# Hashed attention ahead of two feed-forward layers: sign bits laid by DMA below the features of the second score product, scores copied under a ceiling

## What is computed

```python
q_bits = (np.einsum('bhsd,dk->bhsk', q, proj) > 0)
k_bits = (np.einsum('bhsd,dk->bhsk', k, proj) > 0)
mask = q_bucket[:, :, :, None] == k_bucket[:, :, None, :]
scores = np.where(mask, scale * np.matmul(q, k.transpose(0, 1, 3, 2)), -1000000000.0)
attn = np.exp(scores - np.max(scores, axis=-1, keepdims=True))
attn = attn / (np.sum(attn, axis=-1, keepdims=True) + 1e-09)
out = np.matmul(attn, v)
```

## Time and profile before

| | us |
|---|---|
| median of 3 runs | 783.49 (781.36 to 784.22) |
| profiled execution | 782.37 |
| its span, first to last instruction | 780.6 |
| PE busy | 763.5 (98%) |
| DVE busy | 405.1 (52%) |
| ACT busy | 343.6 (44%) |
| POOL busy | 288.9 (37%) |
| granted TensorE clock, mean | 0.999 |

### The profile page before, as it was taken

How to read it: one execution, slowest core, us unless ns; L and a number is a source line. 1 busy time by engine, 2 the same in 40 slices (tenths; PEclk the granted TensorE clock), 3 DMA queues, 4 the chain that set the end, 5 groups by cost and what they waited for, 6 DMA issues and landing times.

```text
span 780.6 us, 12163 instructions
## 1 busy us (share of the span) xinstructions
PE 763.5 (98%) x3800; PEld 644.7 (83%) x3800; DVE 405.1 (52%) x688; ACT 343.6 (44%) x657; POOL 288.9 (37%) x230
## 2 busy tenths in 40 slices
PE   7999999999999999999999999999999999999998
PEld 6788888888889888888888888888888888888886
DVE  5888887888898574343333432352323333242333
ACT  7988898888987221232212322132221312222121
POOL 3688878878897493000000366660000000000000
PEclk9999999999999999999999999999999999999999
DMA  6576667666762342000000032310001000010001
GB/s 168 136 148 167 146 141 177 151 127 157 157 120 61 84 136 82 1 0 1 1 0 1 27 100 89 107 55 0 1 1 42 11 0 0 0 54 0 0 0 54
DMA packets 46312, 52.77 MB, mean 68 GB/s; under 512 B 8912, under 2 KB 34768, under 8 KB 46288
## 3 DMA queue, kind: packets, MB, share of 16 engines
q1 hardware_dynamic: 46064, 52.13, 27.0%
q10 hardware_dynamic: 224, 0.33, 0.2%
HBM read 32.73 MB, written 3.19 MB: 46 GB/s over the span
## 4 chain that ended last, share of the span: by engine, by line
PE 75%; DMA 8%; POOL 6%; issue 5%; SPq 3%; DVE 2%; ACT 0%; POOLq 0%; DVEq 0%
PE acc L594 33%; PE h_ps L576 32%; DMA inv_dram<-row_inv 4%; DMA all_inv<-inv_dram 3%; PE pt_ps L542 2%; POOL wa_lo L431 2%; POOL kt L385 2%; PE pv_ps L556 2%; PE pv_ps L557 1%; PE s_ps L528 1%; PE s_ps L529 1%; POOL wa_hi L429 1%; POOL pt_hi L395 1%; DMA w_raw<-w_out_dram 1%; DVE w_raw L837 1%
## 5 line engine op out<-in xcount | busy, mean ns | idle before, releaser
L770 ACT ACTIVATE r_sb<-h_ps 128x512 f32<-128x512 f32 x96 | 57.4, 598 | 368.0 <-PE h_ps L576 368.0
L909 DVE TENSOR_SCALAR g_sb<-e_sb,sb_scale 128x512 f32<-128x512 f32 x48 | 27.9, 582 | 158.2 <-ACT e_sb L773 158.2
L907 DVE SCALAR_TENSOR_TENSOR g_sb<-e_sb,h_ps 128x512 f32<-128x512 f32 x48 | 33.0, 687 | 135.6 <-ACT e_sb L773 135.1
L804 DVE TENSOR_REDUCE row_min<-s_ps 128x1 f32<-128x768 f32 x96 | 91.5, 954 | 10.3 <-PE s_ps L529 9.6
L693 ACT ACTIVATE probs<-s_ps,row_min 128x768 f32<-128x768 f32 x96 | 87.0, 906 | 11.3 <-DVE row_min L804 9.3
L542 PE MATMUL pt_ps<-cst,probs 128*128 128x128 f32 x576 | 80.8, 275 | 0.7 <-DVE pt_lo L811 0.5
L556 PE MATMUL pv_ps<-pt_hi,v_nat 128*128 128x384 f32 x192 | 72.6, 378 | 7.8 <-DVE w_raw L837 7.7
L576 PE MATMUL h_ps<-xt_hi,wa_lo 128*128 (+1 forms) x192 | 74.7, 389 | 0.0
L576 PE MATMUL h_ps<-xt_lo,wa_hi 128*128 (+1 forms) x192 | 74.7, 389 | 0.0
L576 PE MATMUL h_ps<-xt_hi,wa_hi 128*128 (+1 forms) x192 | 74.7, 389 | 0.0
L576 PE MATMUL h_ps<-xt_hi,wb_hi 128*128 (+1 forms) x192 | 74.7, 389 | 0.0
(11 more groups left out here) (93 smaller groups left out, 1598.3 us busy)
## 6 DMA issues: line engine op xcount, KB each, us to landing
qt<-kt SPq DMA_DIRECT2D x45, 192.0 KB, 3.0
w_raw<-w_in_dram SPq DMA_DIRECT2D x32, 256.0 KB, 2.7
w_raw<-w_out_dram SPq DMA_DIRECT2D x32, 256.0 KB, 2.9
all_inv<-inv_dram SPq DMA_DIRECT2D x32, 192.0 KB, 3.7
raw<-qk_dram SPq DMA_DIRECT2D x15, 384.0 KB, 4.3
raw_v<-v_dram SPq DMA_DIRECT2D x16, 192.0 KB, 4.7
out_dram<-o_sb SPq DMA_DIRECT2D x12, 256.0 KB, 2.1
kt<-kt SPq DMA_DIRECT2D x15, 192.0 KB, 3.7
```

Of the source, the lines that this page charges most:

```text
L804: nc.vector.tensor_reduce(row_min[:, k:k + 1], s_ps[k % 2][:, :, 0:HALF], AX.XY, ALU.min).then_inc(min_done, 1)
```

## The change

- **Bits in place of buckets.** `counts`, `onehot`, `penalty` and the constants for them go. DVE writes the sign bits as 0 or +-2^31, once for q and once for its opposite, and so for k, on 108 partitions (`write_bits`); SP lays them by four DMAs per head in 12 rows below the 64 features of `qt2` and `kt2` (`copy_bits`). The second score product has 76 rows; each bit that differs adds -2^62.
- **Scores copied.** DVE's `keep_scores` takes `row_minimum`'s place: it reads `s_ps`, multiplies by -scale, cuts at a ceiling of 2^56, writes the result to `probs` (now three buffers) and the row's least value beside it. `exp` works in place in `probs`. PE may overwrite a score buffer when it is kept, no longer when its exponential is done. `scale_q` goes.
- **Sums.** POOL adds eps (`add_eps`); DVE only takes the reciprocal, now in the first unit of the next group.
- **Signs of a head** are made at one place (the end of a head's last unit), and `write_bits` follows in the next unit on DVE.
- **Queues.** SP's and POOL's orders change; the copy of q's high part is one DMA with two destinations; only slices 0, 1 (first pair) and 2, 3 (last pair) of the weights are split during attention, the other twelve at the beginning of the layers.
- **Start.** The first head's signs come from an fp32 product on raw data; its parts are made on ACT, DVE and POOL without DMA; 10 instead of 12 idle matmuls keep PE warm.

```diff
             def scores(u, k):
...
-                wait(pe, exp_done, u - 1)
+                wait(pe, scores_kept, u - 1)
                 q1 = qt1[par][:, t * P:(t + 1) * P]
-                q2 = qt2[par][:, t * P:(t + 1) * P]
+                q2 = qt2[par][score_rows, t * P:(t + 1) * P]
...
-            def row_minimum(u, k):
+            def keep_scores(u, k):
+
                 dve.wait_ge(scores_done, u + 1)
-                nc.vector.tensor_reduce(row_min[:, k:k + 1], s_ps[k % 2][:, :, 0:HALF], AX.XY,
-                                        ALU.min).then_inc(min_done, 1)
+                wait(dve, pt_done, 2 * u - 2 * (SRING - 1))
+                ts(probs[k % SRING][:].rearrange("p (n c) -> p n c", n=2), s_ps[k % 2][:, :, 0:HALF], -SCALE, CEILING,
+                   ALU.mult, ALU.min, accum_out=row_min[:, k:k + 1]).then_inc(scores_kept, 1)
...
             def write_bits(head):
-                dve.wait_ge(z_done, head + 1)
-                ts(bits[:], prep_ps[0:SIGN_ROWS, 0:HALF], 0.0, None, ALU.is_gt).then_inc(bits_done, 1)
+                rows = slice(0, SIGN_ROWS)
+                dve.wait_ge(z_done, head)
+                wait(dve, bits_copied, 64 * head - 64)
+                to_bits(bits[:], prep_ps[rows, 0:HALF], rows).then_inc(bits_done, 1)
...
+            def copy_bits(head, par):
+
+                sp.wait_ge(bits_done, head)
+                for n in range(2):
+                    cols = slice(n * HALF, (n + 1) * HALF)
+                    for at, dst in ((n * HALF_ROWS, qt2), (n * HALF_ROWS + K_ROWS, kt2)):
+                        sp.dma_start(dst[par][bit_rows, cols].bitcast(F32),
+                                     bits[at:at + BIT_PAIR, :].bitcast(F32)).then_inc(bits_copied, 16)
...
+            def add_eps(i, g):
+
+                c = slice(g * HT, (g + 1) * HT)
+                pool.wait_ge(exp_done, HT * (GROUPS * i + g) + HT)
+                pool.nop(nofuse=True)
+                nc.gpsimd.tensor_scalar(row_inv[:, c], row_sum[:, c], EPS, 1.0, ALU.add, ALU.mult).then_inc(sum_done, 1)
...
                 if third == 1 and not (first and k < 2 * HT):
                     normalise(i, k // HT - 2)
-                if third == 2:
-                    invert(i, k // HT)
+                if third == 0 and not (first and k == 0):
+                    invert(i, k // HT - 1)
...
-            def pair(i, prev=True, nxt=True):
+            def pair(i, prev=True, nxt=True, weights=()):
                 split_third(i, 0)
-                split_w(at(wa_hi, i), at(wa_lo, i), i, 0, i + 1)
+                add_eps(i, 0)
+                if weights:
+                    split_w(at(wa_hi, weights[0]), at(wa_lo, weights[0]), weights[0], 0, weights[0] + 1)
+                if prev:
+                    split_x(i - 1, 0)
                 if nxt:
                     split_qk(2 * i + 2, 0)
+                add_eps(i, 1)
                 split_third(i, 1)
                 if prev:
-                    split_x(i - 1, 0)
+                    split_x(i - 1, 1)
                 split_third(i, 2)
+                add_eps(i, 2)
                 split_v(2 * i + 1, 1)
```

More of the change, by code:

```diff
@@ L346, in _ @@
             load_qk(2, 0)
-            copy_q(1, 1)
+            copy_q_hi(1, 1)
+            copy_q_lo(1, 1)
             load_qk(3, 1)
             load_w(0, 0, 0, 0)
-            pair(0, prev=False)
+            pair(0, prev=False, weights=(1, 2))
             with sp.Fori(1, PAIRS - 2) as i:
@@ L353, in _ @@
             pair(PAIRS - 2, after=False)
-            pair(PAIRS - 1, nxt=False, after=False)
+            pair(PAIRS - 1, nxt=False, after=False, weights=(3, 4))
             get_inv(PAIRS, -1)
@@ L506, in counts, with first_signs @@
-            def counts(head, n, bank=prep_ps):
-                pe.wait_ge(bits_done, head + 1)
-                rows = slice(n * BIT_ROWS, n * BIT_ROWS + 2 * BITS)
-                mm(bank[:, 0:HALF], code[rows, :], bits[rows, :], start=True, stop=True).then_inc(counts_done, 1)
-            def buckets_out(count):
-                wait(pe, onehot_done, count)
-                wait(pe, penalty_done, count)
+            def first_signs():
+                pe.wait_ge(planes_built, 1)
+                pe.wait_ge(k0_in, 16)
+                pe.wait_ge(q0_in, 16)
+                for n in range(2):
+                    last = mm(s_ps[1][0:HEAD_ROWS, n, 0:HALF], planes[:, 0:HEAD_ROWS],
+                              raw[0][:, n * HALF:(n + 1) * HALF], start=True, stop=True)
+                last.then_inc(z0_done, 1)
@@ new lines, in signs @@
+            def signs(head, par):
+                pe.wait_ge(planes_split, 2)
+                pe.wait_ge(qk_split, head)
+                wait(pe, bits_done, head - 1)
+                dst = prep_ps[0:SIGN_ROWS, 0:HALF]
+                for n in range(2):
+                    cols, plane = slice(n * HALF, (n + 1) * HALF), slice(n * P, n * P + SIGN_ROWS)
+                    mm(dst, planes_hi[:, plane], kt1[par][:, cols], start=n == 0, stop=False)
+                    mm(dst, planes_lo[:, plane], kt1[par][:, cols], start=False, stop=False)
+                    last = mm(dst, planes_hi[:, plane], kt2[par][:, cols], start=False, stop=n == 1)
+                last.then_inc(z_done, 1)
@@ L613, in unit @@
                 transpose_probs(i, u, k, 1)
-                if follows and t == CODE_A:
-                    counts(head, 0)
-                if follows and t == CODE_B:
-                    buckets_out(2 * head + 1)
-                    counts(head, 1)
                 if third == 0 and not (first and k < 2 * HT):
@@ L622, in unit, with first_head @@
                     times_v(i, k // HT - 1, range(2) if third == 1 else range(2, 4))
[L623 to L629 removed]
+                if first and k == 0:
+                    signs(head, par)
+                if more and t == SIGN_UNIT:
+                    signs(head + 1, 1 - par)
+            def first_head(n):
+                pe.wait_ge(q0_hi, 2 * n + 2)
+                pe.wait_ge(q0_lo, n + 1)
+                pe.wait_ge(q0_bits, n + 1)
             pe.wait_ge(zeros_ready, 1)
             keep_warm(WARM)
[L634 to L646 removed]
+            first_signs()
+            keep_warm(WARM_GAP)
+            pe.wait_ge(k0_hi, 2)
+            pe.wait_ge(k0_lo, 1)
+            pe.wait_ge(k0_bits, 1)
+            first_head(0)
+            scores(0, 0)
+            pe.wait_ge(q0_bits, 2)
+            scores(1, 1)
+            pe.wait_ge(ident_in, 16)
             for k in range(UNITS):
@@ L853, in unit @@
                     split_lo(i, u, k, 1)
-                if follows and t in (CODE_A, CODE_B):
-                    penalty(head, par, t - CODE_A)
-                if follows and t == SIGN_B:
-                    write_bits(head)
+                if t == BITS_UNIT and (k < TILES or more):
+                    write_bits(2 * i + k // TILES + 1)
             nc.vector.memset(pt_hi[0][:, 0, :].bitcast(F32), 0.0).then_inc(zeros_ready, 1)
-            nc.vector.memset(row_sum[:, :, 1:2], EPS).then_inc(eps_ready, 1)
@@ L870, in _ @@
[L870 to L879 removed]
+            dve.wait_ge(planes_cleared, 1)
```

368 lines of the change are left out of this document (163 added, 205 removed).

## The result

The changed kernel takes 814.78 us (median of 4 runs, 812.3 to 816.62) beside 783.26 us for the kernel before in the same comparison: a ratio of 1.0403, 95% interval 1.0369 to 1.0438. The forecast was 767 us, the other way. The profiled execution took 816.62 us.

A forecast was written before the change was run, and what follows sets the result against it. PE's work plus counts and waits was taken to bound attention, 30.33 us a pair. Pairs of 28.3 give 14.2 us over seven, plus 1.5 at the start, less 0.4 in the last pair: 15.3 off 782.4, forecast 767, range 754 to 777.

The forecast's parts named there:

- Bits by DMA, and the new queues: SP's and POOL's queues in each pair: later moves cause PE waits of 0.65, 0.45 and about 0.2 us.
- the sum: Time per attention pair: PE's own 26.7 us plus waits 0.65, 0.45, 0.2 and 0.3 make 28.3.
- 0.65 for the signs: PE before the sign products: POOL's `split_qk` ends at 12.85, PE wants it at 12.3; 0.65 us per pair.
- Counts and their shape: PE in attention: dropping the counts, 0.46 us each, takes 1.84 us per pair off PE.
- The copy under a ceiling: DVE's copy of scores from PSUM: 1.0 us taken, range 0.95 to 1.25.
- VectorE is not the bound: Rival: with a score copy of 1.25 us or more DVE sets the pair, 772 to 782 us; chance 0.16.
- the slower rival: PE's 76-row score product costs 0.14 us per change of shape, 6.8 per pair, 809 us in all; chance 0.09.
- The 0.45 a pair for a late sum: DVE waits for POOL's eps sum in the tenth unit, so a multiplication reaches PE 0.45 us late per pair.
- The start: Way to the first exponential: a gain of 1.5 us, between a loss of 1 and a gain of 2.5.
- The last pair: Last attention pair, where POOL also splits two weight slices: a loss of 0.4 us.
- the bound of 1: Layers: no further cost; 1 us if the chain of weight splits there grew by 3 us.
- the title's third part: Reciprocals three to a partition: changes nothing, as the transfer to DRAM already has 1.5 KB, 128 x 3 floats.

The follow-up runs named there:

- e18: Changed kernel with SyncE's reciprocal fetches behind q copies, GpSimd's order largely put back, two second-product buffers, v and first/last-pair weight loads behind the first group's fetch: 774.9 us, 0.9887.
- e1: Changed kernel with SyncE's fetches of the first and third group's reciprocals put back behind the copies of q: 795.2 us, ratio 1.0152.
- e4: Changed kernel with only one of the four copies of bits issued from the third head on (output not the reference's): 799.3 us, ratio 1.0208.
- e13: Kernel before the change, with SyncE's fetches of the first and third group's reciprocals moved ahead of the copies of q: 792.1 us, ratio 1.0040.
- e8: Changed kernel with 26 extra products of constants on TensorE, ahead of its waits for the bits and the product's bank: 811.7 us, ratio 1.0357.

## Why the prediction was wrong

**The step that failed is "Bits by DMA, and the new queues".** It took SyncE as free when the bits are ready (2.45 after the pair's first score product) and priced an issue from the earlier trace rows, 0.52, a copy of 64 rows. Counted from that product:

| | forecast | changed | e18 |
|---|---|---|---|
| copy of k issued | not named | 5.0 | 2.3 |
| first copy of bits | 2.45 | 5.6 | 2.9 |
| last one issued | 4.55 | 8.65 | 5.95 |
| second move issued | 5.6 | 10.15 | 7.4 |

Two things were missing. The diff moves the fetch of the reciprocals ahead of the copies of q; I followed what stood behind the bits and not what now stood in front of the copy of k, where SyncE is held for 2.6 us by the reciprocals' way to memory before it may issue q. And a copy of 12 rows takes 0.71 to 0.80 us to issue, so four take 3.1 instead of 2.1. The landing was forecast at 7.8 and came at 13.0 (VectorE goes on at 126.89): of these 5.2 us, 3.1 stand in front of the first copy of bits, 1.0 is in their issues, 0.45 behind them, and 0.7 is the move's own way (2.9 instead of 2.2). VectorE was not late: the bits are written at 2.6, where 2.45 was forecast. A chain that was to have slack became the longest and closed on itself. e1 (2.8 us a pair), e4 (2.2) and e13 (0.4% without bits) show both halves.

**What waits behind the landing was named only in part.** GpSimd's wait for the moves was forecast and is there, 6.48 us of it. TensorE's was not: the sum has 0.65 for the signs (its own figures, 12.85 and 12.3, give 0.55), and in the changed kernel TensorE never waits for them. It waits for the bits (1.61) and for the bank (2.20), terms that the sum puts at nothing, and runs slow products behind them; the wait for the signs shows only once these are shortened or filled (1.26 in e1, 1.3 in e8). Together that makes 6.8 us of the second group instead of 0.65.

**The rest stood.** Counts and their shape are gone: three units in 6.2 us. The copy under a ceiling lasts 0.956 us and the accumulator read 0.084, 1.04 against 1.0 taken; as the read starts together with VectorE's next instruction, from the copy's start to that one pass only 0.88 (119.00 to 119.88; 0.87 for the reduction before, 117.01 to 117.88). VectorE is not the bound; the Trainium skill's rule (VectorE: DVE Perf Modes, "Two Vector instructions with no wait between them") is seen here in the separate accumulator read. The product over 76 rows starts 0.175 after its neighbours, which refutes the slower rival: the kernel was slower for another reason. The 0.45 a pair for a late sum did not show: VectorE waits 0.3 us in all for it in the changed kernel's pairs, 2.5 in e18's. With the queue mended a pair takes 28.5 us where the sum said 28.3; that is partly luck, since e18 has another order and a buffer more, and TensorE waits there for the bank (4.7 us for `w_raw`, 4.1 for `x_second`, in all pairs) and not for the signs.

**Smaller terms.** The start gave 0.96 at the first copies instead of 1.5. The last pair was to lose 0.4 and lost 6.5, to the same two waits (1.83 and 3.48 there) and slow products behind them (granted clock 0.89 over that pair). The layers lost 3.25, over the bound of 1, nearly all in their first 20 us: TensorE waits 2.02 for `g_lo` there, then starts products 0.43 apart instead of 0.23 for a while (granted clock 0.91 over these 20 us, 1.00 before the change), and gets 75 products done where it did 89. Why `g_lo` came late is not shown. What the prediction calls the title's third part, reciprocals three to a partition, is not in the change: that transfer is the same in both kernels.

## What to carry to other kernels

An in-order DMA queue is an engine: write down its list for one period, with every wait and every issue, and follow it around until it meets itself; a step that is moved is priced by what it now stands in front of. Mend the longest chain first: here GpSimd's order was worth nothing while SyncE's held the loop and 1.2% after it, and a full clock bought waiting time there (in the layers' first 20 us, where TensorE itself is the limit, a low clock did cost time). Price an issue from a transfer of the same shape, not from a larger one.

## What the hardware showed unexpectedly

A small transfer can take longer to issue than a large one: 0.71 to 0.80 us for 12 rows of 1.5 KB (0.73 to 0.74 from ScalarE), against 0.33 to 0.45 for the 192 KB fetch and 0.48 for 64 rows. Bytes alone do not say it, for the 1.5 KB of reciprocals mostly take 0.33 to 0.37; what does is not shown, and now and then an issue of another kind takes longer still (1.33 for one copy of q above). And a granted clock of 0.76 over a group of three units cost 0.3 us in the changed kernel, because what it slowed had to wait for GpSimd anyway: filling the waits with products brought the clock to 1.00 and the time hardly moved.
